# Attention, routed experts and MLP on one core: who swaps the halves of the turned keys

## What is computed

```python
def _attn_ref(q, k, v, tau):            # q, k, v: (4, 8, 576, 64)
    scale = 1.0 / np.sqrt(q.shape[-1])
    scores = scale * np.matmul(q, k.transpose(0, 1, 3, 2))
    thresh = np.max(scores, axis=-1, keepdims=True) - tau
    scores = np.where(scores >= thresh, scores, -1000000000.0)
    scores = scores - np.max(scores, axis=-1, keepdims=True)
    attn = np.exp(scores)
    attn = attn / (np.sum(attn, axis=-1, keepdims=True) + 1e-09)
    return np.matmul(attn, v)

x = attn_out.transpose(0, 2, 1, 3).reshape(2304, 512)
# each row goes to its best expert of 8:  gate * (relu(x @ w1[e]) @ w2[e])
# then an MLP:                            (h * sigmoid(1.702 h)) @ w_out,  h = x @ w_in
```

## Time and profile before

| | |
|---|---|
| median of 3 runs | 1000.06 us |
| the profiled execution | 1000.17 us, span 998.6 us |
| granted TensorE clock, mean | 0.995 of full |
| TensorE busy | 972.2 us, 97% of the span |
| DVE, ScalarE, GpSimd busy | 502.7, 447.3, 256.2 us |
| attention stage | to about 320 us |
| expert stage, then MLP | to about 588 us, then to the end |

### The profile page before, as it was taken

One profiled execution on the slowest core, in us unless ns is written; L12 is line 12 of the kernel. 1 busy time (PEld: TensorE's weight loads), 2 busy tenths in 40 slices (PEclk: granted clock), 3 DMA queues, 4 the chain that ended last, 5 costly groups with the idle time before them and its releaser, 6 DMA issues.

```text
span 998.6 us, 18965 instructions
## 1 busy us (share of the span) xinstructions
PE 972.2 (97%) x6508; PEld 867.1 (87%) x6509; DVE 502.7 (50%) x1142; ACT 447.3 (45%) x1013; POOL 256.2 (26%) x357
## 2 busy tenths in 40 slices
PE   5999999999999999999999999999999999999996
PEld 5778787878787799999999999989999999999995
DVE  6988788888889685212125155522223223222221
ACT  4778787878788514221124154422222222222221
POOL 5655565556565212111112100010010100100101
PEclk8999999999999999999999999999999999999999
DMA  3323222222344118511112542200100101000000
GB/s 62 73 60 72 47 60 65 66 49 61 91 103 130 38 42 255 178 42 42 42 42 79 173 159 64 64 32 1 32 32 0 56 7 32 32 0 0 32 1 32
DMA packets 106904, 61.08 MB, mean 61 GB/s; under 512 B 87373, under 2 KB 95587, under 8 KB 106851
## 3 DMA queue, kind: packets, MB, share of 16 engines
q1 hardware_dynamic: 96195, 44.36, 16.9%
q0 software_dynamic: 4160, 10.51, 3.4%
q10 hardware_dynamic: 6496, 5.54, 1.7%
HBM read 45.68 MB, written 14.70 MB: 60 GB/s over the span
## 4 chain that ended last, share of the span: by engine, by line
PE 92%; DVE 3%; issue 2%; ACT 1%; POOL 1%; DMA 0%; SPq 0%; ACTq 0%; POOLq 0%; DVEq 0%
PE s_ps L1790 20%; PE s_ps L1762 13%; PE s_ps L1628 11%; PE o_ps L1577 9%; PE pt_ps L1520 9%; PE s_ps L1563 8%; PE pt_ps L1762 6%; PE misc L1710 5%; PE o_ps L1710 5%; PE pt_ps L1534 3%; PE misc L1602 1%; PE pt_ps L1620 1%; PE misc L1594 1%; DMA qk<-in_k_dram 0%; ACT probs L1386 0%
## 5 line engine op out<-in xcount | busy, mean ns | idle before, releaser
L1279 DVE TENSOR_TENSOR g<-s_ps,sig 128x384 f32<-128x384 f32 x96 | 53.5, 557 | 277.1 <-ACT sig L1491 277.1
L1491 ACT ACTIVATE sig<-s_ps 128x384 f32<-128x384 f32 x96 | 47.2, 492 | 271.5 <-PE s_ps L1790 271.5
L1091 DVE TENSOR_SCALAR_CACHE_REDUCE scores<-s_ps,taus 128x576 f32<-128x576 f32 x144 | 117.7, 817 | 47.5 <-PE s_ps L1563 30.2
L802 DVE SCALAR_TENSOR_TENSOR probs<-scores,thresh,probs 128x576 f32<-128x576 f32 x144 | 136.6, 950 | 0.0
L1520 PE MATMUL pt_ps<-ident,probs 128*128 128x128 f32 x720 | 127.0, 278 | 3.9 <-ACT pT L1302 1.8
L1790 PE MATMUL s_ps<-yT_high,w_in_high 128*128 (+1 forms) x384 | 129.5, 337 | 0.3 <-issue 0.2
L1790 PE MATMUL s_ps<-yT_high,w_in_low 128*128 (+1 forms) x384 | 129.5, 337 | 0.0
L1790 PE MATMUL s_ps<-yT_low,w_in_high 128*128 (+1 forms) x384 | 128.9, 336 | 0.0
L757 POOL DMA_INDIRECT out_dram<-out_sb,table x18 | 17.8, 989 | 417.7 <-ACT out_sb L1466 414.7
L1386 ACT ACTIVATE probs<-scores,row_low 128x576 f32<-128x576 f32 x144 | 115.4, 801 | 7.5 <-DVE scores L1091 6.1
L1520 PEld LDWEIGHTS pt_ps<-ident,probs 128*128 128x128 f32 x720 | 83.5, 141 | 28.0 <-issue 18.4
(11 more groups left out here) (277 smaller groups left out, 2177.7 us busy)
## 6 DMA issues: line engine op xcount, KB each, us to landing
w_raw<-in_moe_w_dram SPq DMA_DIRECT2D x24, 512.0 KB, 4.6
yT_dram<-tile_yT ACTq DMA_DIRECT2D x10, 512.0 KB, 3.0
x_dram<-xs SPq DMA_DIRECT2D x32, 128.0 KB, 2.2
w_in_raw<-in_moe_w_in_dram SPq DMA_DIRECT2D x4, 1024.0 KB, 5.9
w_out_raw<-in_moe_w_out_dram SPq DMA_DIRECT2D x16, 256.0 KB, 2.6
qk<-in_k_dram SPq DMA_DIRECT2D x30, 128.0 KB, 2.4
next_yT<-yT_dram SPq DMA_DIRECT2D x5, 768.0 KB, 4.4
qk<-in_q_dram SPq DMA_DIRECT2D x16, 128.0 KB, 2.1
```

What stands on the lines that cost most here:

```text
L802: dve.scalar_tensor_tensor(out=probs[:, i % PROB_SLOTS, 0:SEQ], in0=scores[:, i % SCORE_SLOTS], scalar=thresh[:, j, u:u + 1], in1=probs[:, ...
L1091: dve.tensor_scalar(scores[:, i % SCORE_SLOTS].rearrange("p (c n) -> p c n", c=2), s_ps[i % 2][:, :, 0:HALF], taus[:, 3:4], None, ALU.mult ...
```

## The change

The two GpSimd copies of a swap become two transfers from on-chip memory to on-chip memory, issued by ScalarE's queue: each moves 64 partitions x 2304 bytes. Side 1 of a pair is issued at the start of its step u = 0, side 0 of the next pair at the start of u = 5 (TPB = 5), each before that step's copies, and after a wait for ScalarE's own `turned_copied`. GpSimd's waits on its own thresholds and on its own copies go as well. The first pair's side 0 stays with the DVE. There are two semaphores in place of one, each raised by 16 by a transfer.

```diff
-        k_swapped = sem("k_swapped")
+        k_swapped = [sem(f"k_swapped{side}") for side in range(2)]
@@ gpsimd
-            def swap(pair, j, side):
-
-                wait_apart(pool, turned_copied, pair * U + (TPB if side == 0 else U))
-                cols = slice(side * SEQ, (side + 1) * SEQ)
-                done = pair * 4 + side * 2
-                pool.tensor_copy(k_swap[j][0:DH, cols], qkT[j][DH:P, 1, cols]).then_inc(k_swapped, 1)
-                wait_apart(pool, k_swapped, done + 1)
-                pool.tensor_copy(k_swap[j][DH:P, cols], qkT[j][0:DH, 1, cols]).then_inc(k_swapped, 1)
-                wait_apart(pool, k_swapped, done + 2)
@@ gpsimd, step
-                    if u == 1 and on(pair, 0, PAIRS):
-                        wait_apart(pool, thresh_ready, n + 1)
-                        swap(pair, j, 1)
                     if u == 5 and on(pair, 0, PAIRS - 2):
                         split(pair + 2, 0)
-                    if u == 6 and on(pair, 0, PAIRS - 1):
-                        wait_apart(pool, thresh_ready, n + 1)
-                        swap(pair + 1, 1 - j, 0)
@@ vector
-                dve.tensor_copy(k_swap[0][to, 0:SEQ], qkT[0][of, 1, 0:SEQ]).then_inc(k_swapped, 1)
+                dve.tensor_copy(k_swap[0][to, 0:SEQ], qkT[0][of, 1, 0:SEQ]).then_inc(k_swapped[0], 16)
@@ scalar
+            def swap(pair, j, side):
+
+                wait_apart(act, turned_copied, pair * U + (TPB if side == 0 else U))
+                cols = slice(side * SEQ, (side + 1) * SEQ)
+                for to, of in ((slice(0, DH), slice(DH, P)), (slice(DH, P), slice(0, DH))):
+                    act.dma_start(k_swap[j][to, cols].bitcast(F32), qkT[j][of, 1, cols].bitcast(F32)).then_inc(k_swapped[side], 16)
@@ scalar, step
                     if isinstance(quad, int):
                         early_part(quad, i)
+                    if u == 0 and on(pair, 0, PAIRS):
+                        swap(pair, j, 1)
+                    if u == TPB and on(pair, 0, PAIRS - 1):
+                        swap(pair + 1, 1 - j, 0)
                     if u in (2, 6) and on(pair, 1, PAIRS + 1):
@@ tensor, score
                 if u == 0:
-                    wait(pe, k_swapped, (quad * 2 + j) * 4 + 2)
+                    wait(pe, k_swapped[0], (quad * 2 + j + 1) * 32)
                 if u == TAIL:
-                    wait(pe, k_swapped, (quad * 2 + j) * 4 + 4)
+                    wait(pe, k_swapped[1], (quad * 2 + j + 1) * 32)
```

## The result

1015.35 us (median of 4 runs, 1014.04 to 1016.26) against 1000.06 us in the same comparison: ratio 1.0152, interval 1.0139 to 1.0164. The change makes the kernel slower by 15.3 us, where 12.0 was forecast; 1015.35 lies inside the range of 1003 to 1021. The profiled execution took 1016.15 us, its span is 1014.5 us.

A forecast was written before the change was run, and what follows sets the result against it. The prediction took TensorE (97% busy) as the bound, tied to ScalarE at u=0. 15 pairs x 0.83 = 12.5, less 0.5 for a removed wait, gave +12.0 on 1000.06: 1012.0 us, range 1003 to 1021.

The forecast's parts named there:

- The tie at u=0: At u=0 into u=1, TensorE waits for ScalarE's copy of turned probabilities (pT); any delay there delays the end, pairs 1 to 15.
- D = 0.83: Delay of the pT copy at u=0 from two ScalarE issues: 0.83 us a pair, low 0.39, high 1.50.
- u=5 costs 0: At u=5 the issues delay ScalarE's copy by 0.65 us under 2.83 us of value-product cover: 0.
- Landing costs 0: Swap transfers land within 4.6 us, over 3 us before the scores at u=4 and u=0 need them: 0.
- GpSimd's relief is worth 0: Removing GpSimd's half copies gains 0 in the attention pairs; only one early 0.5 us TensorE wait for L663 goes.
- Issues free: Rival: issues don't hold ScalarE, or something hides them; 999.6 us, no measurable change; chance 0.11.
- Queues take turns: Rival: at u=0 each ScalarE issue waits for one of SP's, delay 1.87 us a pair; 1027.6 us; chance 0.04.
- "ScalarE's added time is the whole sum": ScalarE's delay at u=0, 15 x 0.83 = 12.5 us, less 0.5, makes the whole +12.0 us.

The follow-up runs named there:

- e1: Changed kernel with side 1's two transfers issued at u=1 in place of u=0: 1001.27 us, ratio 1.0017.
- e3: Changed kernel with only side 1 transferred by ScalarE at u=0, side 0 copied by GpSimd as before the change: 1012.49 us.
- e4: Changed kernel with only side 0 transferred by ScalarE at u=5, side 1 copied by GpSimd as before the change: 1000.28 us.
- e6: Kernel before, plus two unused 64 x 16 byte transfers issued by ScalarE at u=0 after the wait for its keys copy: 1015.32 us.
- after: The kernel with the change, as profiled, against the kernel before: median 1015.35 us, profiled execution 1016.15 us.
- e7: e1 with SP's gate stores moved behind the loads of pair 12's step: 1000.59 us.
- e12: e1 with side 1's issues at u=1 put behind a wait for the keys copy of u=0: 1007.3 us, ratio 1.0049.
- e8: Kernel before, plus four unused transfers issued by ScalarE at u=0 after the wait for its keys copy: 1056.68 us.
- e11: e8 without the wait for the keys copy, so four unused transfers at u=0 in the kernel before: 1034.41 us.
- e2: Changed kernel with side 1's first transfer issued at u=0 and its second at u=1: 1004.23 us.
- e10: e6 without the wait for the keys copy, so two unused transfers at u=0 in the kernel before: 1004.55 us.

## Why the prediction came out as it did

- **The tie at u=0.** Shown. e1, e3, e4 and e6 each isolate it: move the issues one step and the loss is 1.2 us, leave them alone there and it is 12.4, take away only them and it is 0.2, put two like them there in the kernel before and it is 15.3.
- **D = 0.83.** Right as a mean, 0.835 over eleven pairs, and the closeness is luck: the terms inside it were off in both directions. In the written-out quads the issues started 0.03 after the copy, not 0.12, and two of them took 0.50 + 0.62 = 1.12, not 1.14, which gives 0.72; where an issue of SP's queue ran beside them the second took 0.1 to 0.2 more, and D was 0.80 to 0.93. In the loop with a register the issues started 0.10 after the keys copy and the pT copy came 0.19 to 0.29 after the issues in place of 0.11, which gives 0.88 to 1.05. The forecast had neither the loop's extra instructions nor SP's part. The Trainium skill, Perfetto Trace Analysis, on the HWDGE DMA instruction, has the sequencer free for the next instruction only at the reported end of an issue; the trace agrees, with 0.11 from that end to the next copy.
- **u=5 costs 0.** Right: 0.65 us of idle ScalarE, 2.84 us unchanged on TensorE, e4 at 1.0002.
- **Landing costs 0.** Right for the steady pairs and for all of after: 2.4 us, no wait. The 4.6 us called a safe ceiling was none: two transfers of pair 12 landed after 6.4 and 7.0, and only the slack behind them kept it free. e1, e7 and e12 show that TensorE waits 1 to 6 us for a side 1 that is issued near the gate stores and a step later.
- **GpSimd's relief is worth 0.** Right in the steady pairs: in e1 GpSimd swaps nothing and the pairs take 19.97 as before. The wait of 0.5 us for L663 in pair 1 is gone as forecast; the first pair costs 0.21 in all. The 0.79 that pair 15 gives back is in e8 and e11 too (0.82 and 0.80), where GpSimd still swaps, so it is not this relief; its cause was not looked for. GpSimd is 39.7 us less busy, not 47, as its thresholds (L701) grew from 515 to 552 ns each.
- **Issues free** was wrong as a rival but not empty. Where the wait is already met, an issue goes ahead beside queued work (e2, e10). I had weighed that rule against issues at the kernel's start, which have no queued work ahead of them, so those rows could not test it; what decided was that this issue waits for the copy just before it.
- **Queues take turns** was right as an event and wrong in its price. It had each issue wait for a whole one of SP's, 1.04 us a pair. In after the second issue of u=0 is 0.1 to 0.2 longer in five of fifteen pairs and ends about 0.3 after SP's; once, in place A, it is 1.2 longer. That the one holds the other is read from such ends alone; no run took SP's issues away.
- **"ScalarE's added time is the whole sum"** is the term that was mis-sized: 12.0 forecast, 15.3 measured. Undisturbed pairs and both ends give 11.1 of the profiled run's 16.0; the missing term is some 5 us in pairs 8, 9 and 12. In place A it is a long issue, 2.23 us of idle TensorE and then a lower clock. In place B two engines and SP's queue stop together behind the gate stores. I had costed traffic and the other queue at nothing because their mean was small.

Open: what makes the two issues long together; and what ScalarE and the DVE waited for from 271 to 275 us in after, where the profile says only `remote`. That the stores bring it about is shown for e1 by e7; that the engines stood without their next instructions, as the late packets of the instruction queues in other runs suggest, is not shown. Open too is whether e12's faster group lacks exactly the late transfer, since only a run of the slower group was profiled. No version beats the kernel before; e4 equals it.

## What to carry to other kernels

A transfer issued from a computing engine's queue costs that engine the issue's length, and the page doesn't count it as busy: find the step where that engine has cover before the one that waits for it, and put the issue there. One step's difference was 14 of 15 us here. An issue behind a wait for the engine's own newest result can't be taken early; one whose wait is long met can, by 0.3 to 0.6 us here, about one issue's length.

## What the runs showed of the hardware that was not expected

- Issue length on ScalarE's queue doesn't depend on size: 1.12 us for two of 64 x 16 bytes and for two of 64 x 2304 bytes; four took 2.61. The next copy on ScalarE starts 0.11 after, in the loop with a register 0.19 to 0.29 after.
- The second of two issues on ScalarE's queue was 0.70 to 0.83 us long in place of 0.62 where an issue of SP's queue ran beside it, and ended 0.27 to 0.38 after SP's (five pairs of after); once it took 1.84.
- An idle TensorE of 1.01 us left the clock at 1.00; after 2.65 us (e8) the granted clock was 0.50 over 3 us, and after 2.23 us (after, place A) 0.56. After 2.07 us in e11 it stayed at 1.00. In e8 the clock made up about four tenths of the loss.
- A transfer between on-chip buffers of 144 KB landed in 2.4 us, but in 6.4 to 7.0 when issued seven microseconds behind the stores of 4-byte elements (after), and was there only about 14 us after its issue when issued between them (e12). From 256 to 258 us the DMA engines of e12 were 98% busy at 25 GB/s.
- Beside the same stores single packets of the instruction queues took 3.4 to 6.6 us (five runs), and SP's queue had one issue of 3.0 to 4.6 us in all twelve kernels that have them there.
